# The Fourier stage of an fp32 transformer block folded along channels as well as along tokens

## What is computed

```python
x = attention(q, k, v)                     # (2, 768, 512)
X = np.fft.fft(x, axis=1)
X = np.fft.fft(X, axis=2)
mixed = np.real(X).astype(np.float32)
u = x + mixed
mu = np.mean(u, axis=-1, keepdims=True)
var = np.mean((u - mu) ** 2, axis=-1, keepdims=True)
un = (u - mu) / np.sqrt(var + 1e-06)
ch = np.maximum(un @ w_ch1, 0.0) @ w_ch2
return u + ch                              # goes into the convolution block
```

## Time and profile before

| | us |
|---|---|
| median of 3 runs | 784.91 (783.96 to 788.56) |
| the profiled execution | 781.4 |
| its span on the core | 779.6 |
| last attention work on PE ends, first token transform begins | 300.6, 301.9 |
| token transforms of batch 0, channel transforms of batch 0 | 301.9 to 317.7, 318.9 to 329.4 |
| the same for batch 1 | 329.4 to 343.5, 344.7 to 355.2 |
| transposes of `un` and the way to the MLP | 355.2 to 359.7 |

### The profile page before, as it was taken

One profiled execution on the slowest core, in us unless ns is written; L12 is line 12 of the kernel. 1 busy time (PEld: TensorE's weight loads), 2 busy tenths in 40 slices (PEclk: granted clock), 3 DMA queues, 4 the chain that ended last, 5 costly groups with the idle time before them and its releaser, 6 DMA issues.

```text
span 779.6 us, 10436 instructions
## 1 busy us (share of the span) xinstructions
PE 729.7 (94%) x4001; PEld 648.2 (83%) x4001; DVE 420.5 (54%) x722; ACT 300.0 (38%) x622; POOL 249.2 (32%) x236
## 2 busy tenths in 40 slices
PE   4799999989989998998999999999999989899998
PEld 4699898989988987997888888888888878898886
DVE  3688989888888878667311131113111168884310
ACT  2467667666767775121101111101101136453311
POOL 3456655646446623005720000000014035641000
PEclk9999999999999999999999999999999999999999
DMA  4434445232445303002310000001022051100011
GB/s 141 133 85 110 106 110 142 73 111 70 120 121 150 90 21 109 1 1 81 109 28 0 1 1 1 0 1 55 0 69 94 0 149 41 28 13 28 28 41 54
DMA packets 26865, 49.02 MB, mean 63 GB/s; under 512 B 4032, under 2 KB 11456, under 8 KB 26304
## 3 DMA queue, kind: packets, MB, share of 16 engines
q1 hardware_dynamic: 24368, 39.49, 17.9%
q0 software_dynamic: 2448, 8.87, 3.5%
HBM read 37.33 MB, written 3.15 MB: 52 GB/s over the span
## 4 chain that ended last, share of the span: by engine, by line
PE 73%; DVE 12%; ACT 5%; issue 3%; POOL 3%; DMA 2%; SPq 1%; ACTq 0%; POOLq 0%; DVEq 0%
PE ps L1162 23%; PE ps L1241 17%; PE ps L1320 9%; PE ps L1306 6%; PE ps L1090 5%; PE ps L1076 4%; PE ps L1033 3%; DVE pt_l L731 2%; PE ps L1064 2%; PE ps L1065 2%; ACT prob L536 2%; DVE row_min L724 2%; ACT pt_h L548 2%; DVE mask_n L765 1%; DVE gate L994 1%
## 5 line engine op out<-in xcount | busy, mean ns | idle before, releaser
L928 DVE SCALAR_TENSOR_TENSOR hid_l<-ps,hid_h 128x512 fp32r<-128x512 f32 x48 | 33.2, 691 | 203.3 <-ACT hid_h L632 203.3
L731 DVE TENSOR_TENSOR pt_l<-ps,pt_h 128x384 fp32r<-128x384 f32 x192 | 101.3, 550 | 37.7 <-ACT pt_h L548 37.3
L632 ACT ACTIVATE hid_h<-ps 128x512 fp32r<-128x512 f32 x48 | 28.7, 599 | 226.9 <-PE ps L1162 226.9
L548 ACT ACTIVATE pt_h<-ps 128x384 fp32r<-128x384 f32 x192 | 84.8, 491 | 68.3 <-PE ps L1076 67.6
L1076 PE MATMUL ps<-cst,prob 128*128 128x128 f32 x576 | 84.5, 282 | 15.2 <-ACT prob L536 9.8
L724 DVE TENSOR_REDUCE row_min<-ps 128x1 f32<-128x768 f32 x96 | 90.3, 941 | 11.2 <-PE ps L1065 11.2
L536 ACT ACTIVATE prob<-ps,row_min 128x768 f32<-128x768 f32 x96 | 87.0, 906 | 8.2 <-DVE row_min L724 7.9
L1076 PEld LDWEIGHTS ps<-cst,prob 128*128 128x128 f32 x576 | 65.8, 145 | 27.4 <-ACT prob L536 18.4
L1064 PE MATMUL ps<-k,q 80*128 80x384 f32 x192 | 74.6, 389 | 3.7 <-ACT prob L536 1.5
L1162 PE MATMUL ps<-un_h,w_h 128*128 128x512 f32 x192 | 75.7, 394 | 1.4 <-DVE un_l L922 1.4
L1241 PE MATMUL ps<-w_h,hid_h 128*128 128x512 f32 x192 | 76.0, 396 | 0.0
(11 more groups left out here) (131 smaller groups left out, 1546.5 us busy)
## 6 DMA issues: line engine op xcount, KB each, us to landing
stage<-in_moe_w_ch SPq DMA_DIRECT2D x16, 256.0 KB, 3.4
w_raw<-in_moe_w_ch SPq DMA_DIRECT2D x16, 256.0 KB, 2.6
raw_d<-in_q SPq DMA_DIRECT2D x8, 384.0 KB, 3.7
raw_d<-in_k SPq DMA_DIRECT2D x8, 384.0 KB, 5.6
raw_qk<-in_q SPq DMA_DIRECT2D x16, 192.0 KB, 3.2
raw_qk<-in_k SPq DMA_DIRECT2D x16, 192.0 KB, 3.4
raw_v<-in_v SPq DMA_DIRECT2D x16, 192.0 KB, 2.5
q<-q SPq DMA_DIRECT2D x16, 192.0 KB, 2.9
```

Of the source, the lines that this page charges most:

```text
L548: nc.scalar.activation(pt_h[a][:, R * hf:R * hf + R, (t % R) * P:(t % R + 1) * P], ps[:, 4 + hf, 0:HALF].rearrange("p (j c) -> p j c", j=R ...
L731: nc.vector.tensor_tensor(pt_l[a][part], ps[:, 4 + hf, 0:HALF].rearrange("p (j c) -> p j c", j=R), as_f32(pt_h[a][part]), ALU.subtract).th ...
```

## The change

The channels are folded in the same way as the tokens: channel d and 512 - d are summed for the cosine and subtracted for the sine. Each half then has 256 channels, which is 2 chunks of 128 rather than 4. Channels 0 and 256 have no partner; they become the columns of an edge chunk of their own.

- `both[b]` holds sums (3 tiles, rows EVEN 0..2) and differences (3 tiles) of mirrored tokens over all 512 channels; the first difference tile, which stands for token 384 and its like, is in both halves: EVEN is 4 rows (3 sums and that one), ODD the 3 differences.
- `fold_even` writes columns 1 and 2 (the difference and the sum of channels 0 and 256) and 3.. (the sums of mirrored channels) of `quad`; `fold_odd` the differences. Column 0 of `quad_h` is the low part of column 1, so the edge chunk has high and low part side by side in one stationary tile.
- The token transform has 5 products a batch: m = 0 the edge chunk (7 matmuls, no low part), m = 1, 2 the even ones (2 + 9 matmuls), m = 3, 4 the odd ones (9). Before, it was 8 products.
- The channel transform has 2 chunks for each product; each cosine product has 2 matmuls more, against `ch_h[:, 2*KC]`, which add what channels 0 and 256 give at odd frequencies.
- The pairs and folds are now long instructions: 1536, 512, 1024, 1020 and 765 elements a partition. GpSimd makes all of batch 0 and the differences and the odd fold of batch 1; VectorE makes the sums and the even fold of batch 1. The high and low parts of `quad` are one instruction each of 1028/1024 and 768.
- The low parts of batch 0 leave the end of `head` in attention, where they stood before the last `store_x`.
- `norm` of block 0 goes from VectorE to GpSimd. In batch 1 the order of PE is unit 0, unit 1, transposes, unit R, transposes, unit 2's two halves with transposes between; VectorE's mixes and `store_un` are interleaved to match, two mixes go behind the first `hid_l`. The statistics of batch 0 stand between the low parts of batch 1.
- The table for channels shrinks from 2 x 2064 to 1290 and 1032 elements a partition.

The diff, cut to its core:

```diff
+        un = stage[:, :, :, :].rearrange("p a b c -> p (a b) c")
+        ZS = 2 * KC + 1
+        def un_bank(blk, kt):
+            return 7 if blk == 0 else 2 + kt % 2
         def z_bank(b, m):
-            return m if b == 0 else (7, 2, 3, 6, 0, 1, 4, 5)[m]
+            return m if b == 0 else (7, 0, 2, 3, 6)[m]
+        def fold_even(engine, b):
+            near, far = both[b][:, EVEN, 0], both[b][:, EVEN, MID]
+            engine.tensor_tensor(quad[b][:, EVEN, 1], near, far, ALU.subtract).then_inc(even_done[b], 1)
+            engine.tensor_tensor(quad[b][:, EVEN, 2], near, far, ALU.add).then_inc(even_done[b], 1)
+            engine.tensor_tensor(quad[b][:, EVEN, 3:COLS], both[b][:, EVEN, 1:MID], both[b][:, EVEN, DM - 1:MID:-1],
+                                 ALU.add).then_inc(even_done[b], 1)
+        def fold_odd(engine, b):
+            engine.tensor_tensor(quad[b][:, ODD, 3:COLS], both[b][:, R:2 * R, 1:MID],
+                                 both[b][:, R:2 * R, DM - 1:MID:-1], ALU.subtract).then_inc(odd_done[b], 1)
+        UNIT_ORDER = [(0, 1, 2, R), (0, 1, R, 2)]
+        MIX_ORDER = (0, 3, 1, 2, 4, 5)
...
# GpSimd
-            for j, op in enumerate((ALU.add, ALU.subtract)):
-                for r in range(R):
-                    nc.gpsimd.tensor_tensor(pair[0][:, j, r, :], x[:, 0, r, :], x[:, 0, R + r, :],
-                                            op).then_inc(pair_done, 1)
+            nc.gpsimd.tensor_tensor(both[0][:, 0:R, :], x[:, 0, 0:R, :], x[:, 0, R:2 * R, :],
+                                    ALU.add).then_inc(sum_done[0], 1)
+            differences(0, slice(0, 1))
+            pool.wait_ge(sum_done[0], 1)
+            pool.wait_ge(diff_done[0], 1)
+            fold_even(nc.gpsimd, 0)
...
+            pool.wait_ge(norm_ready, 1)
+            for t in range(TBT):
+                nc.gpsimd.tensor_scalar(un[:, t, :], x[:, 0, t, :], ln[:, t, 6:7], ln[:, t, 10:11],
+                                        ALU.subtract, ALU.mult).then_inc(un_ready, 1)
...
# ScalarE
+            quad_high_part(0, 0)
+            z_high_part(0, 0)
+            quad_high_part(0, 1)
+            z_high_part(0, 1)
+            z_high_part(0, 2)
+            quad_high_part(1, 0)
+            z_high_part(0, 3)
+            z_high_part(0, 4)
+            quad_high_part(1, 1)
...
# VectorE, batch 0 of the mixes and on
+            for m in range(1, 4):
+                z_low_part(1, m)
+                for n in range(2 * m - 2, 2 * m):
+                    statistics(0, n)
             variance(0)
+            z_low_part(1, 4)
+            deviation(0)
+            mix(1, 0)
+            store_un(0, (0,))
+            mix(1, 3)
+            store_un(0, (1, 2, 3))
+            for n in (1, 2):
                 mix(1, n)
...
# TensorE
+            for b in range(B):
+                for m in range(ZS):
+                    transform_tokens(b, m)
+                pe.wait_ge(z_low, ZS * b + KC + 1)
+                if b == 0:
+                    pe.wait_ge(ch_loaded, 32)
+                transform_channels(b, 0, 0)
+                pe.wait_ge(z_low, ZS * b + ZS)
+                transform_channels(b, 0, 1)
+                transform_channels(b, 1, 0)
+                transform_channels(b, 1, 1)
...
+                else:
+                    turn_un(0, 0)
+                    pe.wait_ge(z_swapped, 4)
+                    transform_channels(b, R, 0)
+                    turn_un(0, 1)
+                    pe.wait_ge(u_step, 4 * NT)
+                    transform_channels(b, 2, 0)
+                    turn_un(0, 2)
+                    transform_channels(b, 2, 1)
+                    turn_un(0, 3)
```

254 lines of the change are left out of this document (142 added, 112 removed).

## The result

| | before | changed |
|---|---|---|
| median | 783.29 us (778.95 to 788.56, 20 runs) | 778.48 us (774.02 to 783.47, 20 runs) |
| ratio | | 0.9938, 95% interval 0.9917 to 0.9958 |
| profiled execution, its span | 781.4, 779.6 | 774.28, 772.2 |
| first down-projection starts, from the end of attention's products | 68.29 | 59.45 |
| from the start of the MLP's last matmul to the end of the span | 150.02 | 151.32 |

The kernel is faster by 0.6%, 4.8 us of the medians (3.3 to 6.5). The forecast was 12, at 772.9 in a range of 765.5 to 778, and it gave a change within 1% a chance of 0.10. The new kernel lies within 1% of the old one, and just outside the range.

What follows compares the result with a forecast made beforehand. PE, busy 94% of the span, bounds the kernel: 20.2 us less work, cut by new waits to 13.5, less 1.5 for the clock, gives 12 us. From the median 784.9 that is 772.9 us, range 765.5 to 778.

Steps and rivals of the forecast that it cites:

- What PE loses: Token and channel transforms: 33 and 34 fewer matmuls a batch, 20.2 us less PE work over two batches.
- GpSimd's chain for batch 0: Sums 3.5 us, first difference 1.3, tiny folds, even fold 2.4: done at 298.2, PE starting at 301.0.
- the slower rival: GpSimd's folds read one operand backwards at a multiple of the normal price, on 6.0 us of path; chance 0.05.
- k = 3: GpSimd's mirrored folds at three times their price, which would leave nothing of the 12 us gain.
- The turns: Batch 0: VectorE and GpSimd exclude each other for whole instructions; PE waits 1.7, 2.3, 0.6 and 2.4, 7.0 us in all.
- The first rival: Engines don't exclude each other for so long: batch 1 at 316.2, MLP at 339.3, 765.3 us total; chance 0.15.
- Its sign: VectorE's `quad_l` of 1024 taking 1.2 us while GpSimd works would show the engines don't take turns.
- "GpSimd scales four tiles": Normalising before batch 1's transposes: 0.66 us a tile on GpSimd, four 2.6; PE then waits 0.5.
- The clock: Slow clock behind the PE waits of 2.4 and 2.9 us: together 0 to 4 us, taken as 1.5.
- The second rival: Clock stays at 1.2 GHz for most of the stage, 14 us lost, giving 785; chance 0.10.
- `down(0)` behind `up(0)`: First down-projection starts 7.0 to 8.2 us after the up-projection, since two mixes stand behind the first `hid_l`.
- The sum: Stage gain of 12.7 to 13.9 us at `down(0)`; 13.5 less 1.5 for the clock gives 12 us.

Runs made afterwards that it cites:

- experiment 7: Changed kernel with batch 0's odd differences and odd fold on VectorE instead of GpSimd, and batch 0's last low part ahead of batch 1's: 780.22 us, one execution.
- experiment 8: Changed kernel with GpSimd's long sums, differences and odd folds (these on VectorE too) cut into pieces of 512 or 255: 776.83 us, one execution.
- experiment 3: Changed kernel plus five discarded 128x512 GpSimd scalings, each with another pair of operations, in two sets: 0.70 to 2.08 us each; no kernel time given.
- experiment 4: Changed kernel with GpSimd's four normalised tiles written as multiply-add instead of subtract-multiply: 773.9 us (4 runs), ratio 0.9877 to the kernel before.
- experiment 5: Changed kernel with discarded matmuls in PE's waits, 10 before batch 0's last wait and 30 before the transposes: 773.33 us (6 runs), ratio 0.9872.

## Where the prediction was right, and where it failed

**What PE loses (right).** The counts came as worked out: 134 matmuls fewer are two batches of 33 and 34. The page has PE busy by 14.9 less, not 20.2. In the stage, from the common zero to down, it is 18.9 less. In attention it is 2.7 more and in the convolution 1.3 more, with the same matmuls: the clock fell twice in the changed kernel's trace of attention (0.72 in 156 to 162 and in 228 to 234) and not in that of before.

**GpSimd's chain for batch 0 (right).** Row by row in the changed kernel, GpSimd:

```profile
290.82 3.48 POOL L491 TENSOR_TENSOR both<-x 128x1536 f32<-128x1536 f32 x1 [10.02 <-DVE x L839]
295.98 2.38 POOL L279 TENSOR_TENSOR quad<-both 128x1020 f32<-128x1020 f32 x1
300.78 2.77 POOL L284 TENSOR_TENSOR quad<-both 128x765 f32<-128x765 f32 x1
```

The line through the earlier trace rows gave 3.5 and 2.4. The fold that reads one operand backwards costs what any other does, so the slower rival is refuted: not k = 3 but k = 1. PE's first product came at 300.87 (forecast 301.0).

**The turns (right in kind, off in order).** VectorE's sum of 1536, 1.7 alone by the forecast's reckoning, took 3.38 from 301.78 and its end lies 1.6 behind that of GpSimd's fold at 303.55. A fold of four elements took 1.90. That is what the Trainium skill has (SBUF — State Buffer, "Who interferes with whom"), a lock for the whole instruction, and by that rule the traces agree at these places. The low part of 768 in experiments 7 and 8, which began first and yet stood, isn't explained by it. What the forecast had wrong is who goes first. It let GpSimd's odd fold run ahead of the low part of 1024. In the trace VectorE's low part began at 300.65, 0.13 ahead, took its 1.21, and the fold stood for 0.9. PE's waits behind its first product then were none, 0.9, 0.5 and 2.05 (3.5 in all) instead of 1.7, 2.3, 0.6 and 2.4 (7.0), and batch 1 began 1.7 sooner on the common zero, even with 1.5 for the clock. The first rival (no turns) doesn't hold: it had batch 1 at 316.2, and the rows show the turns. Its sign, a `quad_l` of 1024 at 1.2 while GpSimd works, did appear, but it was a bad sign: the low part had begun first, and GpSimd's fold was the one to stand (2.77, where 1.84 is its price by the earlier trace rows).

**"GpSimd scales four tiles", 0.66 each (the step that failed).** They took 2.07 each, 8.26 in all, on the path. The forecast read the price of a per-partition scaling of 768 elements, which multiplies twice, the second time by 1.0, and scaled it down to 512. But the new instruction subtracts and then multiplies, and on GpSimd that is another price (experiment 3). Put in the quick form (experiment 4), the same instructions took 3.05 and up came at 46.28, where 47.4 was forecast. So this price is what the stage's miss comes down to. The bounds were at fault too. The earlier trace rows is a row of the same engine and opcode, but at 768 elements and with another pair of operations, and the text took it with no upper end. The nearest dearer rows of GpSimd at 512 elements, 1.31 for two inputs, would have put 2.6 more into the range, and still not the 5.7 that it was. The Trainium skill, too, calls one-input work on GpSimd roughly line-rate (GPSIMD Engine Reference, "Engine selection"). The multiply forms at 0.70 agree with that; subtract and multiply at 2.07 does not, and the measurement decides.

**The clock (too low).** Taken were 1.5, from 0 to 4. Measured are 2.4 in the stage (experiment 5) and 1.3 in the convolution, which the text had as "back to back as before". Of the 2.4, 0.9 comes with the long wait for GpSimd. The second rival (the low level for most of the stage) doesn't hold: the granted clock was 1.00 in 302 to 304 and 1.00 again in 318 to 321, behind the first fall, and 0.99 in 345 to 360.

**`down(0)` behind `up(0)` (right).** 7.2, forecast 7.0 to 8.2.

**The sum.** The forecast for the stage was 12.7 to 13.9 ahead of the clock, and 12 with it. The wrong price alone takes 5.3 from that: from `norm_ready` at 335.1, four at 2.07 end at 343.4, where the forecast had the transposes at 338.06. That leaves 6.7. The stage gained 8.8 against the one trace of before and 8.4 against the mean of four, since the waits of batch 0 were 3.5 shorter than forecast, which is more than what the clock took over its 1.5. The last part cost 1.3; that leaves 7.1 to 7.5, near the 7.1 by which the two profiled executions differ. The medians differ by 4.8. Of the other 2.3 to 2.7, 0.2 to 0.3 lies outside the span (device time less span is 1.8 before and 2.0 to 2.1 with the change). The rest, if the untraced runs went as the traced ones, lies in attention, whose end scatters by 8 us. It isn't lost in the last head, beside which the new work of GpSimd begins: from GpSimd's first sum to the end of attention's last product it is 7.77 to 7.80 in the four traces of before and 7.75 to 7.80 in the fourteen with the change. Ahead of that the engines' code is the same. The luck of the 20 runs doesn't explain it alone, since all 77 timed runs of the kernel before have a mean of 783.2 and the 32 of the changed one 778.0. What does stays open.

## What to carry to other kernels

Price an instruction that moves to GpSimd by its pair of operations as well as by its shape. Where no row has that pair, take a bound from the dearest row near it, or write it as multiply-add. When PE's work shrinks, ask for each of its new waits what stands ahead of the releasing instruction on its engine: here three changes of order, one change of engine and a second PSUM bank brought 14 to 15 us of the medians, 12.8 at down in the traces. The change itself, which took 134 of the stage's 328 matmuls away, had brought 4.8 and 8.8. And take several traces from a common zero before a gain of 1% is looked for in one span.

## What the runs showed of the hardware

- GpSimd's `tensor_scalar` on 128x512 fp32: 0.70 to 0.76 us for multiply-multiply and multiply-add, 1.57 for a single subtraction, 1.92 to 2.08 for subtract-multiply, add-add and multiply-subtract, whether the scalars are constants or come from memory.
- A waiting VectorE instruction doesn't get a turn after each of GpSimd's: a low part of 0.95 took 4.8 us beside several of them, cut into pieces (experiment 8) or whole (experiment 7).
- Untouched code can change by 1.2 to 1.6 us through the granted clock: it fell in the convolution in all 14 traces with the change, at one place in ten and at another in four, and in none of the 4 of before, behind waits of the same length.
- The same code can meet the low clock for longer in one trace than in another: 42 matmuls took 7.8 us in one of six traces and 6.7 in the others.
